# A delta-rule attention kernel on one core: the hops' masked matrix held block-diagonal for a pair of heads, as one 128 by 128 product in place of two of 64 by 64

## The reference

```python
def _attn_ref(q, k, v, beta):                 # (4, 8, 768, 48) each, beta (4, 8, 768)
    k_n = k / (np.linalg.norm(k, axis=-1, keepdims=True) + 1e-06)
    state = np.zeros((B, H, D, D), dtype=np.float32)
    for t in range(S):
        kt, vt, bt = (k_n[:, :, t], v[:, :, t], beta[:, :, t, None])
        y[:, :, t] = np.einsum('bhd,bhde->bhe', q[:, :, t], state)
        v_old = np.einsum('bhde,bhd->bhe', state, kt)
        state = state + bt[:, :, :, None] * np.einsum('bhd,bhe->bhde', kt, vt - v_old)
    return y
```

## Time and profile before

| | before |
|---|---|
| median of three runs | 842.01 us |
| the profiled execution | 837.97 us |
| its span, first to last instruction | 836.2 us |
| mean granted clock of TensorE | 0.990 |
| attention: first solve to the last product | about 35 to 267 us of the span |
| TensorE matmuls busy over the span | 779.1 us (93%) |

### The profile page before, as it was taken

One profiled execution on the slowest core, in us unless ns is written; L12 is line 12 of the kernel. 1 busy time (PEld: TensorE's weight loads), 2 busy tenths in 40 slices (PEclk: granted clock), 3 DMA queues, 4 the chain that ended last, 5 costly groups with the idle time before them and its releaser, 6 DMA issues.

```text
span 836.2 us, 24883 instructions
## 1 busy us (share of the span) xinstructions
PE 779.1 (93%) x10976; PEld 549.9 (66%) x10976; DVE 511.4 (61%) x1238; ACT 317.7 (38%) x635; POOL 164.7 (20%) x201
## 2 busy tenths in 40 slices
PE   4688888888889999999999999999999999999998
PEld 3687888788878556555656566656566666666664
DVE  4987687777856884723562346365546767757422
ACT  3465466556542360402131224242332443524211
POOL 2541224231200101300130010003122323323100
PEclk9899899999999999999999999999999999999999
DMA  9033433332121231010001000000000000000101
GB/s 208 25 89 84 124 93 86 79 80 60 43 78 39 62 114 57 1 57 0 30 29 58 0 29 29 2 0 1 1 1 2 3 28 20 29 11 29 38 23 53
DMA packets 44813, 37.54 MB, mean 45 GB/s; under 512 B 27360, under 2 KB 38818, under 8 KB 44706
## 3 DMA queue, kind: packets, MB, share of 16 engines
q1 hardware_dynamic: 37925, 30.90, 12.9%
q10 hardware_dynamic: 6781, 5.05, 2.5%
HBM read 26.50 MB, written 4.72 MB: 37 GB/s over the span
## 4 chain that ended last, share of the span: by engine, by line
PE 81%; DVE 7%; issue 5%; ACT 4%; DMA 2%; SPq 0%; POOL 0%; DVEq 0%; ACTq 0%
PE bank L305 15%; PE bank L1081 6%; PE bank L1129 6%; PE bank L1083 6%; PE bank L1128 6%; PE bank L1127 6%; PE bank L1082 6%; PE bank L1065 5%; PE bank L1067 5%; PE bank L1066 5%; PE bank L337 3%; ACT Dy L443 2%; PE bank L360 2%; PE bank L1105 1%; PE bank L1106 1%
## 5 line engine op out<-in xcount | busy, mean ns | idle before, releaser
L1246 ACT ACTIVATE hT_hi<-bank 128x384 f16<-128x384 f32 x96 | 46.6, 489 | 162.9 <-PE bank L1067 162.9
L1520 DVE SCALAR_TENSOR_TENSOR hT_lo<-bank,hT_hi 128x384 f16<-128x384 f32 x96 | 53.3, 556 | 73.5 <-ACT hT_hi L1246 72.9
L1065 PE MATMUL bank<-unT,wA 128*128 128x384 f16 x288 | 94.0, 326 | 2.1 <-DVE hT_lo L1520 2.1
L1081 PE MATMUL bank<-wA,hT_hi 128*128 128x384 f16 x288 | 94.0, 326 | 1.3 <-DVE hT_lo L1520 1.3
L1067 PE MATMUL bank<-unT,wA 128*128 128x384 f16 x288 | 93.9, 326 | 0.0
L1066 PE MATMUL bank<-unT,wA 128*128 128x384 f16 x288 | 93.9, 326 | 0.0
L1083 PE MATMUL bank<-wA,hT_lo 128*128 128x384 f16 x288 | 93.9, 326 | 0.0
L1082 PE MATMUL bank<-wA,hT_hi 128*128 128x384 f16 x288 | 93.9, 326 | 0.0
L305 PE MATMUL bank<-Yv,ET 64*64 64x48 f32 x2304 | 74.4, 218 | 4.2 <-ACT Yv L443 2.9
L305 PEld LDWEIGHTS bank<-Yv,ET 64*64 64x64 f32 x2304 | 72.2, 135 | 6.8 <-ACT Yv L443 5.0
L443 ACT ACTIVATE Yv<-bank,rows 128x384 f32<-128x384 f32 x72 | 40.5, 577 | 69.5 <-PE bank L305 69.3
(11 more groups left out here) (212 smaller groups left out, 1657.4 us busy)
## 6 DMA issues: line engine op xcount, KB each, us to landing
Kb<-k_dram SPq DMA_DIRECT2D x24, 192.0 KB, 3.7
Vv<-v_dram SPq DMA_DIRECT2D x12, 384.0 KB, 3.8
z_first<-w_dram SPq DMA_DIRECT2D x8, 576.0 KB, 4.0
z_first<-wt_dram SPq DMA_DIRECT2D x8, 576.0 KB, 3.6
out_dram<-hT_hi SPq DMA_DIRECT2D x24, 192.0 KB, 1.9
KQ<-q_dram SPq DMA_DIRECT2D x44, 96.0 KB, 2.3
X<-Yo ACTq DMA_DIRECT2D x12, 192.0 KB
X<-Yo ACTq DMA_DIRECT2D x10, 189.0 KB
```

The costliest lines, as they stand in the source:

```text
L1065: pe.matmul(out, w1[0][:, k, cols], unT[0][:, k, :], start=(k == 0), stop=False)
L1081: pe.matmul(out, hT[0][:, f, cols], w2[0][:, f, :], start=(f == 0), stop=False)
L1520: dve.scalar_tensor_tensor(hT[1][:, f, :], bank[3 + m % 3][:, 0:TG * P], 0.0, hT[0][:, f, :], ALU.max, ALU.subtract).then_inc(s_hl, 1)
```

## The change

ET gets a second column block: for each group it is 128 by 128, with the first head's matrix in its upper left corner and the second head's in the lower right. The other two corners are zeroed once at the start, on VectorE. Each hop issues one product of 128 by 128 by 48 per group. `mask_e` writes two instructions for each bank, one for each half of the partitions, and each leaves out the first 16 columns, which the mask makes zero. KQ takes another place in memory, behind other tiles, and its ring is counted from n + 1.

```diff
-        ET = sb("ET", [P, NG, C])
+        ET = sb("ET", [P, NG, 2, C])
...
-                    "E": (s_et, 2 * n + u + 1), "O": (s_oe, 2 * n + u + 1)}[kind]
+                    "E": (s_et, 4 * n + 2 * u + 2), "O": (s_oe, 2 * n + u + 1)}[kind]
...
-                            sp.dma_start(KQ[feat[r], n % RT, 1, h], A["q"][h, :, n, grp(r)]).then_inc(s_qd[n % RT], 16)
+                            sp.dma_start(KQ[feat[r], (n + 1) % RT, 1, h], A["q"][h, :, n, grp(r)]).then_inc(s_qd[n % RT], 16)
...
                     if k == 1:
-                        pe.wait_ge(s_et, 2 * c + a + 1)
+                        pe.wait_ge(s_et, 4 * c + 2 * a + 2)
                     for j in range(HG):
                         g = a * HG + j
-                        mm = pair(chain(a)[:, j * D:(j + 1) * D], ET[:, g], Yv[:, c % 2, g], False, True)
+                        mm = pe.matmul(chain(a)[:, j * D:(j + 1) * D], ET[:, g].rearrange("p x t -> p (x t)"), Yv[:, c % 2, g],
+                                       start=False, stop=True, skip_group_check=True)
                     mm.then_inc(s_Y, 1)
...
                 if n:
                     dve.wait_ge(s_Y, 8 * n)
-                dve.tensor_tensor(ET[:, grp(u)], ring("E", n, u)[:].rearrange("p (g t) -> p g t", g=HG),
-                                  mE[:].unsqueeze(1).broadcast_to([P, HG, C]), ALU.mult).then_inc(s_et, 1)
+                else:
+                    dve.wait_ge(s_ze, 1)
+                for h in range(2):
+                    dve.tensor_tensor(ET[half[h], grp(u), h, BLK:C],
+                                      ring("E", n, u)[half[h]].rearrange("p (g t) -> p g t", g=HG)[:, :, BLK:C],
+                                      mE[half[h], BLK:C].unsqueeze(1).broadcast_to([C, HG, C - BLK]), ALU.mult).then_inc(s_et, 1)
...
             for a in range(2):
                 dve.memset(state(a), 0.0).then_inc(s_zs, 1)
+            dve.memset(ET[:].rearrange("p g x t -> p (g x t)"), 0.0).then_inc(s_ze, 1)
```

More of the change, by code:

```diff
@@ L99, in attention @@
         Ab, PT = AP[:, :, :, 0], AP[:, :, :, 1]
-        KQ = sb("KQ", [P, RT, 2, 2, HG, C])
         Yo = sb("Yo", [P, 2, NG, D])
         Yv = sb("Yv", [P, 2, NG, D])
-        ET = sb("ET", [P, NG, C])
+        ET = sb("ET", [P, NG, 2, C])
         TT = sb("TT", [P, NG, C])
@@ L115, in attention @@
         cT = sb("cT", [P, 2, 2, BLK])
+        KQ = sb("KQ", [P, RT, 2, 2, HG, C])
         Dy = sb("Dy", [P, BLK, NG, 2])
@@ L128, in attention @@
         s_cst, s_id = sem("tables_loaded"), sem("identity_loaded")
-        s_zk, s_zs = sem("K_zeros"), sem("S_zeros")
+        s_zk, s_zs, s_ze = sem("K_zeros"), sem("S_zeros"), sem("E_zeros")
         s_kd = [sem(f"k_loaded{i}") for i in range(RK)]
@@ L336, in gram @@
                     for h, r in TILES:
-                        mm = pe.matmul(out[r][half[h], j * P:(j + 1) * P], KQ[feat[r], n % RT, 0, h, m],
-                                       KQ[feat[r], n % RT, :, h, m], start=True, stop=True, skip_group_check=True)
+                        mm = pe.matmul(out[r][half[h], j * P:(j + 1) * P], KQ[feat[r], (n + 1) % RT, 0, h, m],
+                                       KQ[feat[r], (n + 1) % RT, :, h, m], start=True, stop=True, skip_group_check=True)
                 mm.then_inc(s_gp, 1)
@@ L359, in predicted @@
                     for h, r in TILES:
-                        mm = pe.matmul(chain(r)[half[h], m * D:(m + 1) * D], KQ[feat[r], c % RT, 0, h, m],
+                        mm = pe.matmul(chain(r)[half[h], m * D:(m + 1) * D], KQ[feat[r], (c + 1) % RT, 0, h, m],
                                        Sv[feat[r], c % 2, h * HG + m], start=m == 0, stop=True, skip_group_check=True)
@@ L393, in queried @@
                         for h, r in TILES:
-                            mm = pe.matmul(out[r][half[h], m], KQ[feat[r], c % RT, 1, h, m], Sv[feat[r], c % 2, h * HG + m],
+                            mm = pe.matmul(out[r][half[h], m], KQ[feat[r], (c + 1) % RT, 1, h, m], Sv[feat[r], c % 2, h * HG + m],
                                            start=m == 0, stop=False, skip_group_check=True)
@@ L459, in turned @@
                     act.wait_ge(s_T, 2 * n + i + 1)
-                    copy(KQ[:, n % RT, 0, :, 4 * i:4 * i + 4].rearrange("p h m t -> p h (m t)"),
+                    copy(KQ[:, (n + 1) % RT, 0, :, 4 * i:4 * i + 4].rearrange("p h m t -> p h (m t)"),
                          ring("T", n, i)[:].rearrange("p (h w) -> p h w", h=2)).then_inc(s_kt, 1)
@@ L530, in _ @@
                 for r in range(2):
-                    act.dma_start(KQ[feat[r], 0, 1, h], A["q"][h, :, 0, grp(r)]).then_inc(s_qd[0], 16)
+                    act.dma_start(KQ[feat[r], 1, 1, h], A["q"][h, :, 0, grp(r)]).then_inc(s_qd[0], 16)
             for src, dst in ((A["mP"], mP[:]), (A["mU"], mU[:]), (A["mE"], mE[:])):
```

## The result

The changed kernel takes 945.29 us, the median of four runs, against 841.92 for the kernel before, of which there are four runs now too: a ratio of 1.112 [1.106, 1.118]. The direction was forecast, the size was not: 896.3 us with a range of 876 to 910. The four runs are far apart, 927.93, 940.66, 949.92 and 976.43 us, and their mean granted clocks over the span go with them: 0.931, 0.924, 0.905 and 0.884. The ratio leaves out the two longest, which are more of the same effect and no disturbance, so it is rather too low. The profiled execution is the shortest, 927.93 us with a span of 926.1; against the span before it is 89.9 us longer.

A forecast was written before the change was run, and what follows sets the result against it. TensorE was taken to bound attention. Hops +60.9, changes of shape +2.8, waits for Yv -2.9 and issue waits -6.5 sum to +54.3 us; against the median of 842.01 that gives 896.3 us, range 876 to 910.

The forecast's parts named there:

- the fourth rival, "The clock": In attention, the new order brings two more stretches of lowered clock: +7 us, 903 us; chance 0.05.
- The hops: In attention's 36 hops, loading 128 columns takes 111.4 ns a record, 3.56 us a hop against 1.87: +60.9 us.
- Changes of shape: Between hops and other products, two ways in and out a chunk instead of one: +2.8 us, bounds 0 and twice that.
- waits for Yv: Ahead of hop 3, TensorE's waits for ScalarE's copies go: -2.9 us, bounds 0 and -3.6.
- The issue waits: In attention, TensorE's waits for arriving code, 26.1 us, shrink by 6.5 us; bounds 0 and -13.
- rival 1: In attention, slow hops fill a store of code and all 26.1 us of issue waits go: 876.7 us; chance 0.13.
- VectorE: Four masks a chunk instead of two, +0.8 us a chunk, and the zeroing at the start, 2.1 us, cost nothing.
- rival 2, faster: In the hops, instruction count or the 48 moving columns set the pace, not the load: -28 us, 814 us; chance 0.04.

The follow-up runs named there:

- e2: The changed kernel with 96 columns moving, 48 of them zeros, in 14 of a hop's 16 products, same loads: 900.01 us, ratio 1.067.
- e8: The changed kernel with its block-diagonal product in hop 1 alone, moving 96 columns, and pairs of products in hops 2 and 3: 868.55 us.
- e3: The kernel before, its hops moving 24 of each group's 48 columns with the same loads: 859.38 us, ratio 1.017.
- e1_layout: The changed kernel with its tile, masks and places, but each hop issues pairs of 64 by 64 products again: 845.45 us, ratio 1.002.
- e5_narrow: The kernel before, with hops 2 and 3 loading only columns 32 to 63 of ET: 843.52 us, ratio 0.999.
- e4: The changed kernel with 0.001 in place of zeros in the two corners beside the diagonal: 949.77 us.
- e2b: The changed kernel with 96 columns moving in its hops, run again with more rounds: 900.13 us, ratio 1.066.

## Why the prediction was wrong

**The step that failed** is the fourth rival, "The clock". It was named, but given 0.05 and +7 us, as two more stretches like the one of the earlier trace rows; the sum itself had nothing for it. The stretch of the earlier trace rows comes at a wait of 2.58 us, so it couldn't tell what the new hops would do, and the prediction never asked what a product that loads 128 columns and moves 48 does to the clock. The runs put in its place: the clock falls in and behind such hops with TensorE busy (seven of nine falls). These falls are gone when 96 columns move at the same pace (e2, e8), and the kernel before gets more falls by moving 24 in place of 48 (e3). The median is 49.0 us over the forecast of 896.3, and 45.2 of them are gone with 96 columns. In the profiled execution 117 us of attention are at 1.2 GHz. The span is 31.7 us longer than that of the second run with 96 columns; the hops are 30.2 us of it in busy time, and the other products of attention are slowed too, while issue gives back: it sums to 22.2 us in that run, and to 10.8 in the changed kernel, perhaps because an array at half pace uses up code more slowly, which no run shows.

In the Trainium skill, TensorE: Matmul & The Clock Gate, HAM oscillation, the rule is to leave TensorE no long idle gaps. The two falls of the kernel before, with waits of 2.58 and 3.10 us beside them, point the same way. But a kernel can keep the rule and fall all the same: 40.00 busy us of 40 at a granted 0.69 in the changed one.

**The hops, right.** 60.9 us were predicted from products with 97 moving columns; with 96 columns and a clock of 0.988 the busy time rose by 59.5. The step of a record in the hops at the full clock is near 113 ns, between the bounds of 109 and 117.

**Changes of shape and waits for Yv, right as far as seen.** In the timeline above gram's last product starts near 155.65 + 1.10 - 0.28 = 156.47 and hop 2 at 156.68, 0.2 us for a way in; no hop waits for Yv any more.

**The issue waits, right as far as a trace can tell.** Predicted 26.1 - 6.5 = 19.6 us; with the clock up it is 22.2 (and 30.5 in e1_layout, whose products are those of the kernel before, so one trace gives this sum to some 4 us). The prediction's rival 1 (a store of code that slow hops fill) wanted them nearly gone, and falls: 8.8 us of them still stand ahead of the products with the state, behind three slow hops. The eight blocks of instructions for TensorE of the Trainium skill (Runtime: NRT & Kernel Launch, Instruction fetch mechanics) don't show here as a reserve.

**VectorE, right:** e1_layout is 0.2% from the kernel before. **The prediction's rival 2, faster,** falls with the first row of the trace; the load sets the pace.

## What to carry to other kernels

Two small products beside each other on the diagonal of the array cost one load of 64 columns; held as one block-diagonal product they cost a load of 128, half of it zeros. Where the load is longer than the moving part, count loaded columns, not instructions. Then look at how many columns move in that time: if a change makes it fewer, price the stretch at 1.2 GHz as a case of its own, and try it with more columns moving, or in one stage alone, before the rest. And before an array product is made shorter, look at what its engine waits for beside it: in e5_narrow the hops were busy 10 us less, and the time didn't move beyond its interval.

## What the runs showed that I had not expected

- Work added can make a kernel faster: 96 moving columns in place of 48, half of them zeros, took the median from 945.29 to 900.13 us. The other way, half of the columns taken out of the kernel before made it 1.7% slower.
- Moving zeros was enough to keep the clock up (e2), and loading 0.001 in place of zeros left it falling (e4). Moving other values than zeros in the added columns wasn't tried.
- At 1.2 GHz a record of the hop took 212 ns against 113. The load of weights slows down with the clock.
- In the traces the falls lie in attention, and two executions of one kernel differ in where: in e2 a slow stretch of 20.5 us at 64.5 us, in e2b none there. The time of the changed kernel spreads over 5% (927.93 to 976.43 us), where the kernel before stays within 0.6% in its four runs beside it; in all its runs on record it lies between 837.78 and 854.07 us. What of the chunk's order decides where a fall begins, and when it ends, stays open.
